# Attention part of a fused kernel: value product with the heads as output rows, two heads side by side, and the high parts of q and k cast by DMA

## What is computed

```
scores = q @ k.T / 8 ; bias = -slope[h] * |i - j| ; keep 0 <= i - j < 128, else -1e9
attn   = exp(scores - max) / (sum + 1e-9) ; x = attn @ v          # (2304, 512)
logits = x @ w_gate ; e = argmax ; x = gate * relu(x @ w1[e]) @ w2[e]
out    = sum_e share[e] * relu(x @ w1_[e]) @ w2_[e]
```

## Time and profile before

| | us |
|---|---|
| median of 3 runs (1215.81 to 1221.4) | 1217.76 |
| the profiled execution's own time | 1216.41 |
| its span, first to last instruction | 1214.8 |
| TensorE busy | 1192.8 (98%) |
| VectorE busy | 726.4 (60%) |
| ScalarE busy | 420.0 (35%) |
| GpSimd busy | 794.2 (65%) |

### The profile page before, as it was taken

How to read it: one execution, slowest core, us unless ns; L and a number is a source line. 1 busy time by engine, 2 the same in 40 slices (tenths; PEclk the granted TensorE clock), 3 DMA queues, 4 the chain that set the end, 5 groups by cost and what they waited for, 6 DMA issues and landing times.

```text
span 1214.8 us, 18910 instructions
## 1 busy us (share of the span) xinstructions
PE 1192.8 (98%) x6446; PEld 1051.0 (87%) x6447; DVE 726.4 (60%) x1600; ACT 420.0 (35%) x766; POOL 794.2 (65%) x527
## 2 busy tenths in 40 slices
PE   8999999999999999999999999999999999999997
PEld 6888887788888888999889999999999999899996
DVE  7876987232222247666666666666666666666664
ACT  5655552111111143333333333333333333333330
POOL 5465685856666766658758776678578676666652
PEclk9998999999999999999999999999999999999999
DMA  7855687988888703212111132121211221111101
GB/s 280 278 199 175 244 310 242 338 308 320 320 319 320 304 27 123 79 53 77 70 70 70 70 122 96 70 87 62 86 70 70 81 92 60 66 68 70 70 35 52
DMA packets 46635, 177.79 MB, mean 146 GB/s; under 512 B 9312, under 2 KB 15584, under 8 KB 30176
## 3 DMA queue, kind: packets, MB, share of 16 engines
q1 hardware_dynamic: 29680, 121.57, 28.0%
q0 software_dynamic: 7520, 43.07, 9.6%
q10 hardware_dynamic: 9360, 12.17, 3.0%
HBM read 157.51 MB, written 19.36 MB: 146 GB/s over the span
## 4 chain that ended last, share of the span: by engine, by line
PE 91%; DVE 3%; POOL 2%; DMA 1%; issue 1%; POOLq 0%; ACT 0%; ACTq 0%; SPq 0%; DVEq 0%
PE ps L1835 33%; PE ps L1778 29%; PE ps L1692 9%; PE ps L1676 9%; PE ps L1599 4%; PE ps L1582 2%; PE ps L1703 1%; PE ps L1570 1%; DVE qk_split L1106 1%; PE ps L1571 1%; PE ps L1613 1%; PE ps L1631 1%; DVE scores_probs L1144 1%; POOL k_lo L569 1%; DMA x_rows<-x_by_expert 1%
## 5 line engine op out<-in xcount | busy, mean ns | idle before, releaser
L1525 DVE SCALAR_TENSOR_TENSOR out_sums<-ps,share_token,out_sums 128x512 f32<-128x512 f32 x270 | 202.4, 750 | 134.5 <-PE ps L1835 133.3
L1835 PE MATMUL ps<-w_hi,h_hi 128*128 128x512 f32 x576 | 226.7, 394 | 0.0
L1835 PE MATMUL ps<-w_hi,h_lo 128*128 128x512 f32 x576 | 226.3, 393 | 0.0
L1778 PE MATMUL ps<-x_hi,w_hi 128*128 128x384 f32 x672 | 224.8, 334 | 1.2 <-DVE h_lo L1509 1.2
L1835 PE MATMUL ps<-w_lo,h_hi 128*128 128x512 f32 x576 | 225.9, 392 | 0.0
L1778 PE MATMUL ps<-x_lo,w_hi 128*128 128x384 f32 x672 | 224.8, 335 | 0.0
L1778 PE MATMUL ps<-x_hi,w_lo 128*128 128x384 f32 x672 | 224.8, 334 | 0.0
L751 POOL TENSOR_TENSOR w_lo<-w_raw,w_hi 128x1024 fp32r<-128x1024 f32 x48 | 115.3, 2403 | 160.6 <-ACT w_hi L1012 160.5
L629 POOL TENSOR_TENSOR w_split<-w_raw,w_split 128x2048 fp32r<-128x2048 f32 x31 | 142.4, 4600 | 63.4 <-DMA w_split<-weights 41.2
L1039 ACT ACTIVATE h_hi<-ps 128x384 fp32r<-128x384 f32 x192 | 90.4, 493 | 206.3 <-DVE ps L1494 152.1
L746 POOL TENSOR_TENSOR w_lo<-w_raw,w_hi 128x1024 fp32r<-128x1024 f32 x48 | 115.9, 2415 | 55.1 <-ACT w_hi L1023 55.0
(11 more groups left out here) (229 smaller groups left out, 1912.4 us busy)
## 6 DMA issues: line engine op xcount, KB each, us to landing
w_raw<-weights SPq DMA_DIRECT2D x80, 1024.0 KB, 4.8
w_split<-weights POOLq DMA_DIRECT2D x32, 1024.0 KB, 8.6
qk_raw<-q_k_turned SPq DMA_DIRECT2D x16, 1152.0 KB, 6.8
v_one<-v_ones SPq DMA_DIRECT2D x16, 365.0 KB, 3.4
y_sorted<-y ACTq DMA_DIRECT2D x20, 256.0 KB, 2.6
x_rows<-x_by_expert ACTq DMA_DIRECT2D x19, 256.0 KB, 4.2
v_t<-v_turned SPq DMA_DIRECT2D x16, 288.0 KB, 7.2
x_by_expert<-zeros SPq DMA_DIRECT2D x16, 260.0 KB, 7.4
```

The lines of the kernel that those rows point to most:

```text
L1525: v.scalar_tensor_tensor(out=a_, in0=ps[:, 4 + t % 3, :], scalar=share_, in1=a_, op0=ALU.mult, op1=ALU.add).then_inc(acc_done, 1)
L1778: last = mm(ps[:, bank, 0:HALF_T], wt[:, w, c * P:(c + 1) * P], xt[:, c, x, :], start=(k == 0), stop=(k == 3 * KC - 1))
L1835: last = mm(ps[:, 4 + t % 3, :], ht[:, f, t * P:(t + 1) * P], wt[:, f, :], start=(k == 0), stop=(k == n - 1))
```

## The change

A duo is now one query tile of both heads of a pair. The value product is turned round: v is the stationary operand (64 columns), the turned probabilities stream (128 columns), and the two heads write rows 0 to 63 and 64 to 127 of one bank, alternating. Their result has the heads' dimensions as rows; VectorE copies it (`copy_heads`), and one new product per duo, `back`, five duos behind, turns it back and multiplies by the gate's weights at once (144 columns streamed: a unit matrix and 16 gate columns). The ones column, `gate_v`, v turned and ScalarE's `copy_vg` go; the sums come from the exponential's own accumulator. Normalising is done for a pair in two parts. The high parts of q and k come for pairs from 2 by a DMA of GpSimd that casts (a third buffer of them), and VectorE's casts go; the raw q loads only 64 rows. All that follows a batch moves one duo later.

```diff
+            def load_qk_hi(p):
+                pool.dma_start(qkh[:, hi_buffer(p)].rearrange("p a h s -> p (a h s)"),
+                               qk[:, bass.ds(p * (4 * S), 4 * S)]).then_inc(qk_hi[hi_buffer(p)], 16)
             def split_qk(p, k):
                 if p == 1:
                     pool.wait_ge(second_hi, 2)
                 else:
-                    pool.wait_ge(qk_hi, (p - 2) * 4 + 2)
+                    pool.wait_ge(scores_ready, (p - 1) * QT)
+                if p + 1 < NP:
+                    load_qk_hi(p + 1)
+                if p > 1:
+                    pool.wait_ge(qk_in[k], raw_loads_of(p))
+                    pool.wait_ge(qk_hi[at], (p + 1) // 3 * 16)
...
# ScalarE, soften(j)
                     ins = a.activation(sp_sb[0:m, slot, 0:w], sp_sb[0:m, slot, 0:w], ACT.Exp,
-                                       bias=low[0:m, slot:slot + 1], scale=-1.0)
+                                       bias=low[0:m, slot:slot + 1], scale=-1.0,
+                                       accum_out=den[0:m, n % 2, t, hd, 0:1])
...
# VectorE
+            def copy_heads(j):
+                m, at = ROWS[j % QT], j % OT_BUFFERS
+                if j >= OT_BUFFERS:
+                    dve.wait_ge(back_done, j - OT_BUFFERS + 1)
+                dve.wait_ge(pv_done, j + 1)
+                v.tensor_copy(ot_sb[:, at, 0:m], ps[:, 4 + j % BANKS, 0:m]).then_inc(heads_copied, 1)
...
             for j in range(DUOS + LAGS):
...
+                if 0 <= j - PV_LAG < DUOS:
+                    copy_heads(j - PV_LAG)
+                for n in pair_due(j, QT + 1):
+                    sum_den(n)
+                    turn_den(n)
+                for n in pair_due(j, BACK_LAG + LOW_TILES):
+                    norm(n, 0)
+                for n in pair_due(j, BACK_LAG + QT):
+                    norm(n, 1)
-                if 1 <= j // QT < NP - 1:
-                    for a_, h_ in SPLIT_AT[j % QT]:
-                        split_hi(j // QT + 1, a_, h_)
...
# TensorE, pv(j)
+                if j >= BANKS:
+                    pe.wait_ge(heads_copied, j - BANKS + 1)
                 blocks = key_blocks(t)
                 for i, (kb, _, w) in enumerate(blocks):
+                    for hd in range(2):
+                        c0, v0 = hd * turned_width(t) + i * m, (kb * 2 + hd) * DH
+                        last = mm(ps[hd * DH:(hd + 1) * DH, 4 + j % BANKS, 0:m], v_sb[0:w, n % 2, v0:v0 + DH],
+                                  pt_sb[0:w, j % SOFT_DUOS, c0:c0 + m], start=(i == 0), stop=(i == len(blocks) - 1))
                 last.then_inc(pv_done, 1)
...
+            def back(j):
...
+                pe.wait_ge(heads_copied, j + 1)
+                mm(ps[0:m, 6 + part, at * BACK:(at + 1) * BACK], ot_sb[:, j % OT_BUFFERS, 0:m],
+                   wb_sb[:, n % PAIRS, :], start=True, stop=True).then_inc(back_done, 1)
             def rank(b):
                 pe.wait_ge(onehot_made, b + 1)
-                pe.wait_ge(vg_copied, min(NP, b * PAIRS + PAIRS + 2))
+                pe.wait_ge(heads_normed, 2 + 2 * min(NP, b * PAIRS + PAIRS + 1))
```

More of the change, by code:

```diff
@@ L248, in build @@
         v_loaded = [sem(f"v_loaded{i}") for i in range(2)]
-        vt_in = [sem(f"vt_in{i}") for i in range(2)]
-        banks_cleared = sem("banks_cleared")
-        vg_done = sem("vg_done")
-        vg_copied = sem("vg_copied")
-        qk_hi = sem("qk_hi")
+        back_ident = sem("back_ident")
+        den_set = sem("den_set")
+        heads_copied = sem("heads_copied")
+        back_done = sem("back_done")
+        qk_hi = [sem(f"qk_hi{i}") for i in range(3)]
         first_k = sem("first_k")
@@ L404, in x_bank @@
         def x_bank(i):
-            return 6 if isinstance(i, int) and i == 0 else 4
+            return 2 if isinstance(i, int) and i == 0 else 4
         def second_early(i):
@@ L422, in batch_due, with pair_due @@
         def batch_due(j, after):
-            at = j - (QT * PAIRS + PV_LAG) - after
+            at = j - (QT * PAIRS + BACK_LAG) - after
             b = at // (QT * PAIRS)
             return [b] if at % (QT * PAIRS) == 0 and 0 <= b < B else []
-        def head_due(j):
-            return [h for h in range(HEADS) if (h * QT + QT - 1) // 2 + PV_LAG + 1 == j]
+        def pair_due(j, duo):
+            n = (j - duo) // QT
+            return [n] if (j - duo) % QT == 0 and 0 <= n < NP else []
         @block.sync
@@ new lines, in sum_den, with turn_den, norm @@
+            def sum_den(n):
+                dve.wait_ge(probs_ready, n * QT + QT)
+                if n > 0:
+                    dve.wait_ge(den_turned, n)
+                v.tensor_reduce(den_sum[:], den[:, n % 2], AX.X, ALU.add).then_inc(den_summed, 1)
+            def turn_den(n):
+                dve.wait_ge(den_summed, n + 1)
+                dve.wait_ge(heads_normed, 2 * n)
+                v.reciprocal(rden[:, n % 2], den_sum[:]).then_inc(den_turned, 1)
+            def norm(n, part):
+                first, end = ((0, LOW_TILES), (LOW_TILES, QT))[part]
+                nt = end - first
+                b, p = divmod(n, PAIRS)
+                dve.wait_ge(den_turned, n + 1)
+                dve.wait_ge(back_done, n * QT + end)
+                x = ps[:, 6 + part, 0:nt * BACK].rearrange("p (t e) -> p t e", e=BACK)
+                d = rden[:, n % 2, first:end]
+                v.tensor_tensor(lg_sb[:, 2 * p:2 * p + 2, first:end].rearrange("p h t e -> p t h e"),
+                                x[:, :, P:BACK].rearrange("p t (h e) -> p t h e", h=2),
+                                d.unsqueeze(3).broadcast_to([P, nt, 2, E1]), ALU.mult)
+                v.tensor_tensor(x_sb[:, b * QT + first:b * QT + end, p * P:(p + 1) * P]
+                                .rearrange("p t (h e) -> p t h e", h=2),
+                                x[:, :, 0:P].rearrange("p t (h e) -> p t h e", h=2),
+                                d.unsqueeze(3).broadcast_to([P, nt, 2, DH]), ALU.mult).then_inc(heads_normed, 1)
@@ L1329, in _ @@
             for j in range(DUOS + LAGS):
-                heads = head_due(j)
-                for h in heads:
-                    norm_sum(h)
                 if j < DUOS:
@@ L1635, in _ @@
                 mm(ps[:, 0, 0:2 * P], ident[:], mask[:], start=True, stop=True)
-            pe.wait_ge(gate_in, 16)
-            pe.wait_ge(banks_cleared, 1)
-            for t in range(QT):
-                gate_v(0, t)
             for j in range(DUOS + LAGS):
@@ L1650, in _ @@
                     pv(j - PV_LAG)
+                if 0 <= j - BACK_LAG < DUOS:
+                    back(j - BACK_LAG)
                 for b in batch_due(j, 5):
```

244 lines of the change are left out of this document (103 added, 141 removed).

## The result

The changed kernel takes 1230.46 us (median of 16 runs, 1222.6 to 1236.75) against 1217.95 (16 runs) of the kernel before on the same chip: ratio 1.010, 95% interval 1.0085 to 1.0115. The forecast was 1206.5, the range 1197 to 1224: the measured time lies above it. The profiled execution took 1232.2, its span 1230.6.

A forecast was written before the change was run, and what follows sets the result against it. Attention was taken to be bound by TensorE's passes, next by GpSimd's chain. Pairs of 8.4 us plus chain, load and clock terms end attention at 176.2, 11.1 us earlier than 187.3, giving 1206.5 us; range 1197 to 1224.

The forecast's parts named there:

- Passes of TensorE: Attention on TensorE: the two heads' pv passes run side by side, so a pair takes 8.4 us, not 10.44.
- (a): Attention on TensorE: the heads run one behind the other, a pair takes 10.1 us, 1220 us in all; chance 0.24.
- (b): Attention on TensorE: each change of head empties the array, a pair takes 12.2 us, 1245 us in all; chance 0.09.
- VectorE and `back`: Attention: VectorE falls from 8.54 to about 6.6 us a pair, no bound; back's copy wait uncovered only at end, 0.7 us.
- The clock: Attention: 3.4 us of half clock behind pair 8, and 3 us more for new idle places at pairs 12 and 13.
- GpSimd's chain: Attention: pairs 6 to 8 take 23.2 us, 10 to 12 20.1, 11 to 13 22.5, each against 16.8 for TensorE.
- Loads: Attention: a pair with zeros moves 3.5 MB in 10.1 us, so pair 6 starts at 64, not 59.6.
- Rival (c): Attention: heads side by side but data late, pairs 3 to 6 and 13 to 15 wait 1 to 2 us: 1213; chance 0.15.
- Rival (d): High parts of q and k: the casting DMA alone brings nothing, as nobody waited for VectorE; no chance given.
- ScalarE and ranks: Attention: exponentials' accumulator 1.0 us a pair, beside TensorE; rank waits about 0.8 us, three times, 2.4 us.
- What follows … moves whole: After attention: the rest waits only on what attention releases, so the 11.1 us gain carries through whole.
- The last addition: Final sum: 1216.41 - 11.1 = 1205.3 for a profile, the median of runs 1.35 higher, given as 1206.5 us.

The follow-up runs named there:

- e8_back_between: Changed kernel with the product back issued between the two key blocks of pv, same work: 1248.68 us, ratio 1.0234.
- e11_pieces: Changed kernel with each of GpSimd's two subtractions for a pair cut into four pieces, each waited for: 1220.33 us, ratio 1.0037.
- e2_cast_only: Kernel before with the high parts of q and k by the casting DMA and nothing else: 1216.41 us, ratio 1.0009.
- e1_turned_only: Changed kernel with the high parts of q and k cast by VectorE as before: 1242.53 us, ratio 1.0207.
- e10_warm: Changed kernel with eight useless products before TensorE's waits at pairs 8 and 12: 1225.91 us, ratio 1.0078.
- e16_pieces_v_first: Changed kernel: subtractions from pair 6 but 9 and expert's first in pieces, the latter after pair 15's, scatters a pair later, last v load first: 1218.16 us.
- e13_best: Changed kernel: pieces for six pairs, scatters a pair later, expert's subtraction after the last pair's, v first, first two expert loads behind pair 14: 1223.49 us.
- e14_best_scat: As e13_best, but the expert's first high-part load behind pair 13 and the next two behind pair 14: 1219.37 us, ratio 1.0030.

## Why the prediction was wrong, step by step

**Passes of TensorE.** Right in kind: side by side, rivals (a) and (b) fall. The starts of the two heads' passes lie 6 to 7 ns apart (36.388 and 36.395), and eight pv passes take 0.59 us. For the return from the column halves to the full array I counted nothing, and it costs 0.29 us (`e8_back_between`), 1.4 us a pair with one in each duo. The pair took 8.97 us against my 8.4, so 0.9 of it was made up by other terms; which ones, no run shows. The row I relied on was one 64-column tile next to a 128-column one, with no second half in use, and I carried it over to a use of the array that it did not show. How much of the 0.29 us is TensorE running empty and how much a weight load that nothing hides, the runs do not part.

**VectorE and `back`: the step that failed.** I wrote that `back` is "covered while VectorE is less than about a duo late", put 0.7 us of uncovered wait into the sum, summed VectorE to 6.6 us a pair (6.1 to 6.3 measured) and called it no bound. The load was about right and the conclusion wrong: TensorE waited for the copies seven times, 13.9 us in all. Not VectorE's load counted here, but the longest single instruction in its queue, 7.21 us. Up to pair 13 the sum was 5 us short (it starts at 144.2, forecast 139.1). From there to the mixture it was 13 us short (49.9 us, forecast 34.1 and 3 for the clock), and the 6.4 us wait behind `mark` and the half clock after it lie in that part. The trace of before had the warning: `mark`, 40 columns, took 1.33 us in three batches, and I did not ask what ran beside it. `e11_pieces` shows the cause, `e2_cast_only` that it was there before, and `e1_turned_only` that a busier VectorE makes it worse.

**The clock.** The sum held 3.4 us behind pair 8, half of the 6.70 us at a granted clock of 0.50 in the kernel before, and 3 more. There were 37.5 us at 0.50 from 80 to 250 us, some 6 of which TensorE was idle anyway: (37.5 - 6) / 2 is 16 us lost by this count (a transpose of 128 columns took 0.21 us from start to start at 0.50, at 186.9 us, and 0.11 at 1.00, at 173.6). (One more stretch, 6.8 us from 10.8, lies in the first pairs and is left out.) It is the second mis-sized term, and in part a result of the first, since the longest stretch fell into the wait for a copy. Each of the idle 2.0 us ahead of pairs 8 and 12 was followed by a stretch of 6.8 us, 3.4 us by the same count. `e10_warm` shows that not all of it is a loss: behind pair 12 GpSimd's chain takes the time that the clock gives back.

**GpSimd's chain.** Right: from pair 6 to 8 it took 21.6 us (forecast 23.2), from 10 to 12 21.4 (20.1), from 11 to 13 23.4 (22.5). Idle time ahead of pairs 8 and 12 had the second subtraction as releaser, 2.0 us each, against 6.4 and 3 to 6: less because TensorE took longer than 8.4 us for each pair. With VectorE out of the way the chain is the first in the list (4.6 and 3.7 us in `e11_pieces`).

**Loads.** Rival (c) was part of it: the casting load took 9.0 us in the median to land, and GpSimd waited for it and for raw data, 6.1 and 4.5 us. TensorE's only waits for GpSimd's low parts were those at pairs 8 and 12.

**The casts.** Rival (d) held: `e2_cast_only` is within 0.1%. For the turned product they are worth 12 us (`e1_turned_only`).

**ScalarE and ranks.** The accumulator's read is a row of its own, 187 ns for 128 rows, ten a pair, 1.9 us against my 1.0; hidden, as said. The rank waits were 0.5 us each, three times, where I had put 0.8.

**"What follows … moves whole".** Wrong in both directions. The mixture took 7.8 us longer in the changed kernel, and in `e16_pieces_v_first` it waited for rows, since they hang on the routing's chain and not on TensorE. There, with most holds gone, this step kept most of the forecast gain from the result: 5.9 us of wait and 6.0 of longer mixture out of 14.

**The last addition.** 1205.3 + 1.35 is 1206.7, not 1206.5; nothing hangs on it.

## What to carry to other kernels

Before a product is made to depend on a copy of another engine a few steps old, look at that engine's longest instruction (7.21 us here), not at its load (6.1 to 6.3 us of a pair's 9), and ask of each short operation with a long row what ran beside it. If GpSimd computes beside VectorE's operations on SBUF, cut GpSimd's work into pieces with a wait between: in `e11_pieces` the step that had taken 2.66 us in the median took 0.83. Do it only where somebody waits for VectorE: in the kernel before the same cut cost 5 us. Use column halves in long blocks, since each visit cost 0.29 us here (`e8_back_between`), and follow a gain past the end of its stage: what is next there may hang on another chain.

## What the runs showed of the hardware

- Some of VectorE's operations stand still while GpSimd subtracts: one with two inputs in SBUF took 7.21 us instead of 0.19, over two GpSimd instructions issued back to back; with a wait between pieces the longest such step took 0.84 us (`e11_pieces`). A plain copy of 40 columns from SBUF to SBUF was held too (3.94 us in `e2_cast_only`). A reduction of one SBUF tensor (0.18 us) and masks and copies from PSUM (0.29 and 0.28 us) ran beside a subtraction as usual.
- Two 128x64 products in the two column halves start 6 to 7 ns apart and run together, eight passes in 0.59 us; entering and leaving the halves cost 0.29 us (`e8_back_between`).
- Eight useless products in idle time kept the granted clock at 1.00 where it had been 0.50 for 6.8 us (`e10_warm`). At one of the two places another wait took the time back.
- The same instructions up to pair 13 gave a 4.8 us wait in one execution and 0.3 us in another (`e13_best`, `e14_best_scat`).
